# MLP stage of a token mixer: the last 64 channels of two batches transposed as one block, and copied to both halves of the partitions afterwards

## The reference, cut to what matters

```python
u = x1 + real(fft(fft(x1, seq), channels))        # x1 is the output of a short attention convolution
un = (u - mean(u)) / sqrt(var(u) + 1e-6)          # over the 192 channels of a token
x2 = u + maximum(un @ w_ch1, 0) @ w_ch2           # 192 -> 768 -> 192: the MLP
theta = x2 @ w_theta                              # 192 -> 192
zr, zi = x2 * cos(theta), x2 * sin(theta)
y = w_tok_r @ zr + w_tok_i @ zi                   # over the 4224 tokens
out = (x2 + y) + maximum((x2 + y) @ w_ch, 0)
```

## Time and profile before

| | |
|---|---|
| runs, median (lowest to highest) | 3148.22 us (3147.73 to 3152.39), 3 runs |
| the profiled execution, its own time | 3150.33 us |
| its span in the profile | 3148.5 us |
| mean granted TensorE clock | 0.989 of full speed |
| TensorE busy over the span | 3039.9 us, 97% |
| MLP stage (440 to 1030 us): TensorE, VectorE, ScalarE, GpSimd busy | 580.8, 448.4, 385.3, 386.9 us of 590 |

### The profile page before, as it was taken

One profiled execution on the slowest core, in us unless ns is written; L12 is line 12 of the kernel. 1 busy time (PEld: TensorE's weight loads), 2 busy tenths in 40 slices (PEclk: granted clock), 3 DMA queues, 4 the chain that ended last, 5 costly groups with the idle time before them and its releaser, 6 DMA issues.

```text
span 3148.5 us, 57324 instructions
## 1 busy us (share of the span) xinstructions
PE 3039.9 (97%) x17542; PEld 2873.3 (91%) x17542; DVE 2445.8 (78%) x4263; ACT 1323.5 (42%) x2474; POOL 1635.5 (52%) x1536
## 2 busy tenths in 40 slices
PE   6888889999999899999999999999999999999999
PEld 4666469989898899999999999999999999999999
DVE  8887667777778787878878787887878787887776
ACT  2222346666666443433334333433433343333443
POOL 7897026766667554545445453545545454543221
PEclk9999999999999999999999999999999999999999
DMA  7775742332333666666666565665656666565442
GB/s 246 272 279 194 263 148 101 113 115 101 116 111 121 218 228 218 237 216 226 228 219 233 204 241 208 229 237 212 234 205 238 217 231 224 221 230 172 133 150 65
DMA packets 213450, 618.45 MB, mean 196 GB/s; under 512 B 20288, under 2 KB 61504, under 8 KB 211200
## 3 DMA queue, kind: packets, MB, share of 16 engines
q1 hardware_dynamic: 203600, 603.19, 53.9%
q10 hardware_dynamic: 9696, 13.37, 1.5%
HBM read 399.82 MB, written 216.66 MB: 196 GB/s over the span
## 4 chain that ended last, share of the span: by engine, by line
PE 84%; POOLq 6%; DVE 3%; issue 2%; DMA 1%; POOL 1%; SPq 1%; ACT 1%; DVEq 0%; ACTq 0%
PE banks L1657 63%; PE banks L1485 11%; POOLq L1078 6%; PE banks L1595 4%; PE banks L1597 3%; PE banks L1581 2%; POOL head L1076 1%; PE banks L1734 1%; DMA m_scr<-mst 1%; DVE zl L835 0%; DVE hl L810 0%; SPq L467 0%; PE banks L1571 0%; DVE wl L830 0%; PE banks L1573 0%
## 5 line engine op out<-in xcount | busy, mean ns | idle before, releaser
L1657 PE MATMUL banks<-zh,wh 128*128 128x384 f32 x3828 | 1286.9, 336 | 13.3 <-DVE rbuf L887 13.3
L1657 PE MATMUL banks<-zh,wl 128*128 128x384 f32 x3828 | 1280.7, 335 | 0.0
L1657 PE MATMUL banks<-zl,wh 128*128 128x384 f32 x3828 | 1280.5, 334 | 0.0
L887 DVE TENSOR_TENSOR rbuf<-rbuf,banks 128x384 f32<-128x384 f32 x1168 | 646.2, 553 | 312.1 <-PE banks L1657 274.2
L1657 PEld LDWEIGHTS banks<-zh,wh 128*128 128x128 f32 x3828 | 719.9, 188 | 14.5 <-DVE wl L830 7.3
L1657 PEld LDWEIGHTS banks<-zl,wh 128*128 128x128 f32 x3828 | 719.9, 188 | 0.0
L1657 PEld LDWEIGHTS banks<-zh,wl 128*128 128x128 f32 x3828 | 719.5, 188 | 0.0
L1111 POOL TENSOR_TENSOR wsum<-wraw 128x384 f32<-128x384 f32 x176 | 179.6, 1021 | 1021.0 <-DVE wl L830 895.8
L1302 ACT ACTIVATE wh<-wsum 128x384 fp32r<-128x384 f32 x704 | 370.8, 527 | 722.9 <-PE banks L1657 701.5
L1302 ACT ACTIVATE wh<-wraw 128x384 fp32r<-128x384 f32 x528 | 278.5, 528 | 492.8 <-PE banks L1657 492.8
L830 DVE TENSOR_TENSOR wl<-wsum,wh 128x384 fp32r<-128x384 f32 x664 | 446.0, 672 | 34.3 <-ACT wh L1302 5.1
(11 more groups left out here) (147 smaller groups left out, 4276.7 us busy)
## 6 DMA issues: line engine op xcount, KB each, us to landing
wraw<-w_pairs SPq DMA_DIRECT2D x176, 768.0 KB, 6.7
rbuf<-y_scr SPq DMA_DIRECT2D x176, 768.0 KB, 5.7
y_scr<-rbuf SPq DMA_DIRECT2D x160, 768.0 KB, 4.0
xin<-x_pad SPq DMA_DIRECT2D x22, 1728.0 KB, 8.1
z_scr<-zsc SPq DMA_DIRECT2D x33, 768.0 KB, 4.1
zraw<-z_scr SPq DMA_DIRECT2D x33, 768.0 KB, 7.2
x_scr<-x1s SPq DMA_DIRECT2D x22, 576.0 KB, 3.0
t_scr<-tst ACTq DMA_DIRECT2D x44, 288.0 KB, 4.3
```

The source lines that it names most:

```text
L887: dve.tensor_tensor(part, part, dst(k, i), ALU.add).then_inc(r_done, 1)
L1657: last = pe.matmul(dst, l[w][:, q, :], r[par][:, operand, q, :], start=starts and q == 0 and t == 0, stop=q == 2 and t == 2, skip_group_ch ...
```

## The change

In place of a copy of the rest beside itself, the rest of all 4 batches is packed into one tile of 4 x 64 columns (`un_rest`, `x2_rest`), by one activation of the same size. Two transposes are enough then: the first gives batch 0 in partitions 0 to 63 and batch 1 in 64 to 127, the second batches 2 and 3. Bank 1 is filled to 256 columns. Since the matmuls behind it want each batch's rest in both halves of the partitions, the high part is made by four activations and the low part by four subtractions: for each half of bank 1 (e) and each half of the target (r), one over 64 partitions x 2 x 128 columns. The matmuls and their operands are the same as before. The diff, without the renamed semaphores and tiles:

```diff
+        def both_in(e):
+            return bank[1][D2 * e:D2 * e + D2, 0:2 * P].rearrange("p (j t) -> p j t", j=2)
+
+        def both_out(t, r, e):
+            return t[D2 * r:D2 * r + D2].rearrange("p (j e t) -> p j e t", j=2, e=2)[:, :, e, :]
...
+            def low_both(lo, hi):
+                for e in range(2):
+                    for r in range(2):
+                        last = dve.tensor_tensor(both_out(lo, r, e), both_in(e), f32(both_out(hi, e, e)), ALU.subtract)
+                return last
+
             def low_y(n, i):
                 dve.wait_ge(yh_ready, 2 * n - 1 + i)
-                dve.tensor_tensor((yl1, yl2)[i][:], bank[i][:], f32((yh1, yh2)[i][:]), ALU.subtract).then_inc(yl_ready, 1)
+                if i:
+                    low_both(yl2, yh2).then_inc(yl_ready, 1)
+                else:
+                    dve.tensor_tensor(yl1[:], bank[0][:], f32(yh1[:]), ALU.subtract).then_inc(yl_ready, 1)
...
-                    dve.tensor_tensor(ul2[:], bank[1][:], f32(uh2[:]), ALU.subtract).then_inc(ul_ready, 1)
+                    low_both(ul2, uh2).then_inc(ul_ready, 1)
...
-            def twice_x2(n):
+            def rest_of_x2(n):
                 act.wait_ge(x2_ready, n)
-                act.activation(x2s[:, :, D:D + D2], x2s[:, :, P:D], ACT.Copy).then_inc(x2_twice, 1)
+                wait(act, xt_ready, 2 * n - 2)
+                act.activation(x2_rest[:].rearrange("p (b r) -> p b r", b=B), x2s[:, :, P:D],
+                               ACT.Copy).then_inc(x2r_ready, 1)
+
+            def high_both(t):
+                for e in range(2):
+                    for r in range(2):
+                        last = act.activation(both_out(t, r, e), both_in(e), ACT.Copy)
+                return last
...
                     if live(n + 1) and k == 3:
                         act.wait_ge(un_ready, n + 2)
-                        act.activation(un[:, :, D:D + D2], un[:, :, P:D], ACT.Copy).then_inc(un_twice, 1)
+                        wait(act, ut_ready, n + 1)
+                        act.activation(un_rest[:].rearrange("p (b r) -> p b r", b=B), un[:, :, P:D],
+                                       ACT.Copy).then_inc(rest_ready, 1)
...
-                    act.activation(uh2[:], bank[1][:], ACT.Copy).then_inc(uh_ready, 1)
+                    high_both(uh2).then_inc(uh_ready, 1)
...
+            def rest_transposed(src):
+                for j in range(2):
+                    last = pe.transpose(bank[1][:, P * j:P * j + P], src[:, P * j:P * j + P], idn[:])
                 return last
...
-                    transposed(un, 1).then_inc(ut_ready, 1)
+                    rest_transposed(un_rest).then_inc(ut_ready, 1)
```

More of the change, by code:

```diff
@@ L192, in token_fourier_mixer @@
         mbuf = alloc(C, "mbuf", [P, BD])
-        un = alloc(C, "un", [P, B, D + D2])
+        un = alloc(C, "un", [P, B, D])
+        un_rest = alloc(C, "un_rest", [P, B * D2])
         uh1 = alloc(C, "uh1", [P, B * P], F32R)
@@ L204, in token_fourier_mixer @@
         hl = alloc(C, "hl", [P, HB, B * P], F32R)
-        x2s = alloc(C, "x2s", [P, B, D + D2])
+        x2s = alloc(C, "x2s", [P, B, D])
+        x2_rest = alloc(C, "x2_rest", [P, B * D2])
         yh1 = alloc(C, "yh1", [P, B * P], F32R)
@@ L244, in token_fourier_mixer @@
         cw_in, cwh_ready, cwl_ready = sem("cw_in"), sem("cwh_ready"), sem("cwl_ready")
-        m_in, u_ready, un_ready, un_twice = sem("m_in"), sem("u_ready"), sem("un_ready"), sem("un_twice")
+        m_in, u_ready, un_ready, rest_ready = sem("m_in"), sem("u_ready"), sem("un_ready"), sem("rest_ready")
         seed_ready, rstd_ready = sem("seed_ready"), sem("rstd_ready")
@@ L802, in add_x2 @@
                     wait(dve, x2_kept, m)
-                part = x2s[:, 2 * i:2 * i + 2, 0:D]
+                part = x2s[:, 2 * i:2 * i + 2, :]
                 dve.tensor_tensor(part, tile(s)[:, 2 * i:2 * i + 2, :], banks[:, 4 + 2 * i:6 + 2 * i, D:2 * D], ALU.add)
@@ L1268, in _ @@
             act.wait_ge(s_halfpi, 1)
-            def twice_x2(n):
+            def rest_of_x2(n):
                 act.wait_ge(x2_ready, n)
-                act.activation(x2s[:, :, D:D + D2], x2s[:, :, P:D], ACT.Copy).then_inc(x2_twice, 1)
+                wait(act, xt_ready, 2 * n - 2)
[6 more added lines that the diff above has]
+                return last
             def high_y(n, i):
                 act.wait_ge(xt_ready, 2 * n - 1 + i)
-                act.activation((yh1, yh2)[i][:], bank[i][:], ACT.Copy).then_inc(yh_ready, 1)
+                if i:
+                    high_both(yh2).then_inc(yh_ready, 1)
+                else:
+                    act.activation(yh1[:], bank[0][:], ACT.Copy).then_inc(yh_ready, 1)
             def keep_x2(s):
-                act.activation(tile(s - 1)[:], x2s[:, :, 0:D], ACT.Copy).then_inc(x2_kept, 1)
+                act.activation(tile(s - 1)[:], x2s[:], ACT.Copy).then_inc(x2_kept, 1)
             def keep_theta(n):
@@ L1317, in step_c @@
                     if live(n - 1) and k == 0:
-                        twice_x2(n)
+                        rest_of_x2(n)
                     if live(n - 1) and k in (1, 2):
@@ L1345, in step_c @@
                     for b in range(B):
-                        last = act.activation(un[:, b, 0:D], tile(s + 2)[:, b, :], ACT.Identity, bias=shift_u[:, b:b + 1],
+                        last = act.activation(un[:, b, :], tile(s + 2)[:, b, :], ACT.Identity, bias=shift_u[:, b:b + 1],
                                               scale=rstd[:, b:b + 1])
@@ L1390, in _ @@
             run_c(step_c, act, 0)
-            twice_x2(NT)
+            rest_of_x2(NT)
             high_w(0, 0, 0, 0, 3)
@@ L1577, in _, with transposed @@
             pe.wait_ge(cwl_ready, 5)
-            def transposed(src, part):
+            def transposed(src):
                 for b in range(B):
-                    last = pe.transpose(bank[part][:, P * b:P * b + P], src[:, b, P * part:P * part + P], idn[:])
+                    last = pe.transpose(bank[0][:, P * b:P * b + P], src[:, b, 0:P], idn[:])
+                return last
+            def rest_transposed(src):
+                for j in range(2):
+                    last = pe.transpose(bank[1][:, P * j:P * j + P], src[:, P * j:P * j + P], idn[:])
                 return last
@@ L1601, in transpose_x2 @@
             def transpose_x2(n, i):
-                pe.wait_ge(x2_twice if i else x2_ready, n)
-                transposed(x2s, i).then_inc(xt_ready, 1)
+                pe.wait_ge(x2r_ready if i else x2_ready, n)
+                (rest_transposed(x2_rest) if i else transposed(x2s)).then_inc(xt_ready, 1)
             def theta_product(n):
@@ L1634, in step_c @@
                         pe.wait_ge(m_ready, 4 * NGB - 3)
-                    transposed(un, 0)
+                    transposed(un)
                 if live(n):
@@ L1638, in step_c @@
                 if live(n + 1):
-                    pe.wait_ge(un_twice, n + 2)
+                    pe.wait_ge(rest_ready, n + 2)
                     wait(pe, yl_ready, 2 * n)
-                    transposed(un, 1).then_inc(ut_ready, 1)
+                    rest_transposed(un_rest).then_inc(ut_ready, 1)
                 if live(n - 1):
```

2 lines of the change are left out of this document (1 added, 1 removed).

## The result

| | before | after |
|---|---|---|
| runs, median (lowest to highest) | 3149.68 us (3147.73 to 3152.39), 4 runs | 3202.16 us (3199.82 to 3204.03), 4 runs |
| ratio, with its 95% interval | | 1.0166 (1.0154 to 1.0178) |
| the profiled execution, its span | 3150.33, 3148.5 us | 3199.82, 3198.0 us |
| cadence of an undisturbed step | 17.79 us | 19.07 us |

The account below looks back on a forecast made before the run. The prediction took TensorE as the bound before, a ring of VectorE and ScalarE after. +34.2 (laps), -0.4 (first step), -2.0 (turns), +6.7 (tail) make +38.5, 3186 us; own range 3178 to 3196, 8 in 10 within 3162 to 3202.

Parts of the forecast that it names:

- the ring: MLP step: VectorE's first hl to last angle operation, ScalarE's sines, un, next hh; 16.77 us before, 19.01 after.
- Four subtractions: VectorE's yl2 and ul2: no overlap and no gap, 1.72 us for 0.60, +2.24 a step; chance 0.64.
- rival 1: VectorE's four subtractions overlap like all neighbours, 0.35 us each: lap 18.37, +18.6 us, 3167; chance 0.17.
- the 28 laps: MLP stage, step 2's first hl to step 30's: each lap 19.01 us instead of 17.79, +34.2 us.
- ScalarE's four are covered: ScalarE's yh2 and uh2: four activations add 0.65 us each time but finish before VectorE needs them.
- TensorE 0.42 us a step shorter: TensorE's queue in an MLP step: four fewer transposes, 17.37 us instead of 17.79.
- The turns: Two turns of the MLP loop: waiting TensorE gives back 1.0 us each, -2.0; VectorE's 0.39 stays.
- sign (f): In the changed kernel's trace, the step around the loop's turn is under 1 us longer than the others.
- The tail: Last three steps and start of the token product: six VectorE operations become four each, 6 x 1.12 = +6.7 us.
- The first step: Step 1 of the MLP stage, before the ring closes, runs at TensorE's pace: -0.4 us.
- the one with a drain's spacing: VectorE's four subtractions follow like drained ones, 0.52 us each: lap 19.73, +60.8 us, 3209; chance 0.07.
- the ring does not bind: MLP step: a lap stays under TensorE's 17.37 us, the transposes' 13.9 us are saved, 3134; chance 0.07.

Follow-up runs that it names:

- e1: Changed kernel with VectorE's four subtractions made one over 128 x 512 in yl2 and ul2 (half the low parts from another batch): 3143.18 us, ratio 0.998.
- e4: Kernel before, with yl2 and ul2 each as four subtractions over 64 x 256, in the changed kernel's partition order: 3197.99 us, ratio 1.0154.
- e9: Kernel before, with yl2 and ul2 each as four subtractions, two in the lower half of the partitions, then two in the upper: 3182.12 us, ratio 1.01.
- e2: Changed kernel with ScalarE's four activations made one over 128 x 512 in yh2 and uh2 (half the high parts from another batch): 3203.59 us, ratio 1.0171.
- e7: Changed kernel with VectorE's angle operations put ahead of ul1 and ul2: 3167.33 us, ratio 1.0057.
- e10: Changed kernel with the packed form kept for un's rest alone, x2's rest as before the change: 3230.70 us, ratio 1.0261.
- e12: Changed kernel with only un's rest packed and VectorE's angle operations ahead of un's low subtractions, except in the last three steps: 3158.26 us, ratio 1.0027.
- e6: Changed kernel with GpSimd's sum of u made to wait until the step's last angle operation is done: 3199.93 us, ratio 1.0162.
- e7b: Kernel before, with VectorE's angle operations put ahead of ul1 and ul2: 3152.84 us, ratio 1.0012.

## Why the prediction was right, and where it was short

- **The bound, the ring.** Right. The prediction said that the ring "by itself needs 17.79 - 1.02 = 16.77 us". 16.77 + 2 x 1.14 is 19.05, measured 19.07. In e1, where the ring is short again, the step is 17.35, and in e4 TensorE's four transposes more change nothing.
- **Four subtractions, "0.43 each and 1.72 for four".** Right in kind and nearly in size: 1.73 and 1.75. The two ends that were weighed (1.40 and 2.08) are out. The 0.43 was reckoned from operations of 128 partitions; one of 64 x 256 lasts 0.42. The prediction is wrong in that nowhere in the trace of before an operation starts at another partition than the one before it: behind `wcl` (2867.00 us, 128 x 192, 0.360 long) comes `wcs[D2:P]` (2867.37, 64 x 192 from partition 64 on, 0.355 long), and the next operation at 2867.76. So 64 partitions took as long as 128 there, and the starts are 0.37 and 0.39 us apart, without overlap. That one place spoke for the value between, and against "every undrained pair" of rival 1; e4 and e9 show the same with 1.75 and 1.55 us for the four. The lap of 19.01 is 19.07, the 28 laps are +36 us instead of +34.2.
- **ScalarE's four are covered.** Right for the change (e2), at 0.39 us each, where the sum had 0.28 and allowed for 0.41. It is a statement about this order: with the angle ahead (e7) or with x2's rest left as it was (e10), VectorE waits for them by 0.22 and 0.47 us.
- **TensorE 0.42 us a step shorter.** Right: 17.35 in e1, 17.57 with half of it in e12.
- **The turns, "1.0 back each, -2.0".** This is the step that failed: the irregular steps are +8 us in place of -2.0. The reasoning on the one stop of TensorE held: in e4, which has only that stop, a turn is 0.5 and 0.9 over a step, where the prediction lets 0.39 stay. But the changed kernel's TensorE stops a second time, 1.50 us in the middle of `mlp_up`, where the hidden pieces that the ring needs are made; its turns are 2.7 over a step, so 2.3 together over those of before in place of -2.0, and its sign (f), a turn under 1 us longer than the other steps, did not come. Beside that, the sum put two things at nothing: the meeting of the last angle operation with GpSimd's sum behind each turn (1.6 us each, which e6 took away), and VectorE's pauses of 0.22 to 0.44 us (0.4 in each of these two steps, 1.7 in five others). The three make up the 10 us. In the trace of the kernel before GpSimd's sum starts 1.26 us behind the operation, and pauses of this size stand only at the turns; whether the waits covered more of them there, or the new code brings them, isn't shown. Why TensorE stops a second time stays open.
- **The tail, +6.7.** Near: the last four laps are +8.5, and +7.2 in e4, which has the subtractions alone. But they are +4.1 in e1, which has everything else, so not all of the 8.5 is the six operations; what the rest is stays open. The first step, -0.4, was +0.3.
- **The rivals.** The sum with overlap (3167) and the one with a drain's spacing (3209) are refuted by the 0.43 between starts, "the ring does not bind" by the cadence. The time moved towards the drained rival for another reason: it is outside the forecast's own 3178 to 3196, and 0.16 us above 3202, the upper end of the wide range.

So the lap was worked out well, and what went wrong is what the sum took for regular: a disturbance that the new code brings of its own, and small ones that the old order of the engines kept apart or covered.

## What to carry to other kernels

When a change makes another engine's ring the bound, list what its slack may have covered until now (pauses whose cause the trace doesn't show, a neighbour's operation that came just late enough, a stop at the loop's turn) and charge it in full; here that was 8 of some 50 us. A packed operand that has to be unpacked into both halves of the partitions is paid for on the engine that unpacks; both how many instructions that takes (e1: 59 us back with one for four) and where they stand in the queue (e7: 34 of 52 us back by moving them) decide the price. And try the parts of a change singly before believing that half of it costs half: e10 cost more than the whole.

## What of the hardware was not expected

- A change of partitions between neighbours on VectorE costs 0.10 us here: 1.75 us for the four in e4, 1.55 in e9, with two changes fewer.
- An angle operation of VectorE that sets off 0.06 to 0.10 us behind GpSimd's sum of 128 x 768 takes 1.6 us more: the last one 2.16 (changed kernel) and 2.18 (e10) for 0.56, the first one 2.55 for 0.96 (e10). The x2 sum of 128 x 384, 0.01 us behind it in the changed kernel (753.13), takes its 0.56. A cadence can lock into this: e10 pays it in nearly each step.
- A turn of the loop stops TensorE once in the kernel before, e4, e7b and e9 (1.0 to 1.5 us), but twice in the changed kernel and in e1, e6, e7, e10 and e12 (the second 0.8 to 3.6 us); e2 has two stops at the first turn and a single one of 2.62 us at the second. Which kernels have more than the one short stop goes with the packed transposes in TensorE's code; what sets its length was not tried and stays open.
- Behind TensorE's stops of 2.62 to 3.57 us at the turns (e2, e10, e12) the granted clock was 0.50; behind those up to 1.71 us (e6) it stayed at 1.00.
